# Normalising the attention weights before they are transposed, in a fused attention, gated-layer and expert kernel

## What is computed

```python
scores = scale * np.matmul(q, k.transpose(0, 1, 3, 2))
kth = np.partition(scores, -32, axis=-1)[..., -32:-31]
scores = np.where(scores >= kth, scores, -1e9)
scores = scores - np.max(scores, axis=-1, keepdims=True)
attn = np.exp(scores)
attn = attn / (np.sum(attn, axis=-1, keepdims=True) + 1e-09)
x = (attn @ v) as rows of 8 heads * 64            # 1152 x 512
rms = np.sqrt(np.mean(x * x, axis=-1, keepdims=True) + 1e-06)
xn = x / rms * rms_g
g = xn @ w_gate                                   # 512 x 1536
h = (g * sigmoid(g) * (xn @ w_val)) @ w_out       # 1536 x 512
# then top-1 of 8 experts by h @ gate, each expert relu(h @ w1) @ w2, times its probability
```

## Time and profile before

| what | value |
|---|---|
| median of 3 runs | 645.54 us (644.76 to 645.86) |
| the profiled execution, its own time | 645.43 us |
| its span, first to last instruction | 643.5 us |
| PE busy | 615.3 us |
| DVE busy | 411.7 us |
| ACT busy | 327.1 us |
| POOL busy | 264.4 us |
| mean granted TensorE clock | 0.994 |

### The profile page before, as it was taken

The page is one execution under the profiler, slowest core; times in us unless marked ns, Lnnn a source line. Parts: engine busy times, 40 slices in busy tenths (PEclk is TensorE's granted clock), DMA queues, the critical chain, the costliest instruction groups (busy, mean ns, idle before and its releaser), DMA issues.

```text
span 643.5 us, 11169 instructions
## 1 busy us (share of the span) xinstructions
PE 615.3 (96%) x3954; PEld 475.0 (74%) x3954; DVE 411.7 (64%) x912; ACT 327.1 (51%) x713; POOL 264.4 (41%) x366
## 2 busy tenths in 40 slices
PE   6789989999999999999999999999999999999994
PEld 5465765775765866766766766757589999999994
DVE  4999999898998997997997997902011111011110
ACT  4777876766766766766756757743111111111100
POOL 1876774364465464553654554542310110111101
PEclk9899999999999999999999999999999999999998
DMA  9998800000000000000000000000595876766501
GB/s 241 250 380 303 221 3 0 18 18 2 17 18 1 18 18 2 16 18 2 18 18 2 1 18 2 1 17 1 197 381 175 281 251 214 281 205 248 173 2 39
DMA packets 55182, 65.45 MB, mean 102 GB/s; under 512 B 32282, under 2 KB 32282, under 8 KB 55132
## 3 DMA queue, kind: packets, MB, share of 16 engines
q1 hardware_dynamic: 53388, 60.05, 29.5%
q0 software_dynamic: 1744, 4.76, 2.0%
HBM read 52.89 MB, written 12.30 MB: 101 GB/s over the span
## 4 chain that ended last, share of the span: by engine, by line
PE 85%; DVE 7%; ACT 2%; issue 2%; POOL 1%; DMA 1%; SPq 0%; POOLq 0%; ACTq 0%; DVEq 0%
PE ps L570 14%; PE ps L861 11%; PE ps L847 11%; PE ps L524 7%; PE ps L530 7%; PE ps L525 7%; PE ps L505 6%; PE ps L478 5%; PE ps L463 4%; PE ps L489 4%; DVE w_top L1360 2%; DVE m L1354 2%; PE ps L698 1%; DVE w_top L1347 1%; PE ps L872 1%
## 5 line engine op out<-in xcount | busy, mean ns | idle before, releaser
L1548 POOL TENSOR_TENSOR s_ring<-s_ring,z_pair 128x576 f32<-128x576 f32 x72 | 101.0, 1424 | 62.2 <-ACT z_pair L1055 62.2
L1360 DVE MATCH_REPLACE8 w_top<-m,w_top 128x576 f32<-128x576 f32 x144 | 105.9, 743 | 0.0
L1354 DVE MAX8 m<-w_top 128x8 f32<-128x576 f32 x144 | 101.7, 748 | 0.0
L570 PE MATMUL ps<-wo_space,hid 128*128 128x512 f32 x216 | 100.7, 593 | 0.8 <-issue 0.8
L524 PE MATMUL ps<-w_parts,x_hi 128*128 128x512 f32 x196 | 81.7, 417 | 0.0
L525 PE MATMUL ps<-w_parts,x_hi 128*128 128x512 f32 x196 | 77.4, 395 | 0.0
L861 PE MATMUL ps<-arena,w_loads 128*128 128x168 f32 x512 | 75.8, 307 | 0.5 <-issue 0.5
L1571 POOL DMA_INDIRECT out_rows<-arena,s_ring x16 | 15.1, 944 | 147.0 <-DVE arena L1384 144.6
L847 PE MATMUL ps<-arena,w_loads 128*128 128x168 f32 x512 | 74.3, 306 | 0.6 <-ACT arena L920 0.6
L847 PEld LDWEIGHTS ps<-arena,w_loads 128*128 128x128 f32 x512 | 73.3, 190 | 0.9 <-ACT arena L920 0.9
L861 PEld LDWEIGHTS ps<-arena,w_loads 128*128 128x128 f32 x512 | 73.2, 190 | 0.6 <-issue 0.6
(11 more groups left out here) (142 smaller groups left out, 885.8 us busy)
## 6 DMA issues: line engine op xcount, KB each, us to landing
w_loads<-in_moe_w SPq DMA_DIRECT2D x16, 2048.0 KB, 9.0
dispatched_rows<-drow SPq DMA_DIRECT2D x18, 260.0 KB, 6.7
w_loads<-in_moe_w_gate SPq DMA_DIRECT2D x3, 1024.0 KB, 5.9
w_loads<-in_moe_w_val SPq DMA_DIRECT2D x3, 1024.0 KB, 8.1
wo_space<-in_moe_w_out SPq DMA_DIRECT2D x1, 3072.0 KB, 12.1
arena<-dispatched_rows SPq DMA_DIRECT2D x8, 341.2 KB
out_rows<-drow SPq DMA_DIRECT2D x9, 256.0 KB, 5.4
q_space<-in_q SPq DMA_DIRECT2D x8, 256.0 KB, 4.2
```

The source lines that it names most:

```text
L570: last = mm(blk[0], hid[:, c * P:(c + 1) * P], wo_s[:, c, :], start=(c == 0), stop=(c == CF - 1))
L1354: vec.max(m8[:, 2 * (n % 2) + a, i, :], w_top[:, a, :]).then_inc(s["top_step"], 1)
L1360: vec.match_replace(w_top[:, a, :], m8[:, 2 * (n % 2) + a, i, :], w_top[:, a, :], NEG).then_inc(s["top_step"], 1)
L1548: gp.tensor_tensor(row, row, z_pair[:, a, :], ALU.subtract).then_inc(s["lowered"], 1)
```

## The change

The exponentials are divided by their row sum before PE transposes them. For that each half of a group gets its own two POOL instructions on one value per row (`divide`: add the epsilon, raise to the power -1), followed by an ACT pass over the 576 exponentials (`shares`), and PE's `turn_probs` waits for `shared` in place of `masked`. The product with the values then is x's columns already. So `x_hi` and `x_lo` are made from `oT` (the last pair's `x_hi` straight from PSUM, `last_columns`), the eight transposes around `xrow` with their copies and scalings go, and one turn of four transposes (`turn_columns`) takes their place, which feeds the sum of squares alone. The order on ACT and POOL changes with it: both `probs` of a group stand together in most slots, and from group 11 on (`early_marks`) the marks are made at the end of the slot before, ahead of that slot's last layer work.

```diff
             turned("rk", due(n, ALPHA, RANK))
+            turned("sq", due(n, ALPHA, XB))
             turned("q", next_tile(n))
...
-            turned("xa", due(n, GAMMA, XA))
-            turned("xn", due(n, GAMMA, XA))
...
             def turn_probs(g, a):
-                pe.wait_ge(s["masked"], 2 * g + a + 1)
+                pe.wait_ge(s["shared"], 2 * g + a + 1)
...
             def block_low(t, w_hi, bank):
-                pe.wait_ge(s["t_free"], use["xn", t] + 1)
+                pe.wait_ge(s["x_lo_set"], t + 1)
...
+            def turn_columns(t):
+                pe.wait_ge(s["o_copied"], HP * (t + 1))
+                turn(use["sq", t], lambda c: oT[:, c, :])
...
-                nc.scalar.activation(sqr, xrow[:], ACT.Square,
-                                     scale=float(DM) ** -0.5, accum_out=ssq[:, 0:1]).then_inc(s["x_sum"], 1)
+                nc.scalar.activation(sqr, tb, ACT.Square,
+                                     scale=float(DM) ** -0.5, accum_out=ssq[:, 0:1]).then_inc(s["t_free"], 1)
...
+            def last_columns(t):
+                act.wait_ge(s["pv_done"], H * (t + 1))
+                nc.scalar.activation(x_hi[:, (HP - 1) * P:HP * P], oT_ps, ACT.Copy,
+                                     scale=gain[:, HP - 1:HP]).then_inc(s["x_hi_set"], 1)
...
+            def shares(g, a):
+                act.wait_ge(s["share_set"], 2 * g + a + 1)
+                row = s_ring[:, g % SR, a, :]
+                nc.scalar.activation(row, row, ACT.Copy, scale=rden[:, g % 2, a:a + 1]).then_inc(s["shared"], 1)
...
+            def early_marks(g):
+                return g > FIRST + HP
...
+                if n + 1 <= NG and early_marks(n):
+                    marks(n, 0)
+                    marks(n, 1)
+                t = due(n, GAMMA, XA)
+                if t is not None and t > 0:
+                    columns(t, range(HP - 1))
+                dense(n, GAMMA)
...
+            def divide(g, a):
+                pool.wait_ge(s["masked"], 2 * g + a + 1)
+                gp.tensor_scalar(rden[:, g % 2, a:a + 1], den[:, g % 2, a:a + 1], EPS_SUM, None, ALU.add).then_inc(s["den_step"], 1)
+                pool.wait_ge(s["den_step"], 2 * g + a + 1)
+                gp.tensor_tensor(rden[:, g % 2, a:a + 1], rden[:, g % 2, a:a + 1], nones[:, 0:1], ALU.pow).then_inc(s["share_set"], 1)
...
                         gp.tensor_tensor(row, row, z_pair[:, a, :], ALU.subtract).then_inc(s["lowered"], 1)
+                    divide(g, 0)
+                    divide(g, 1)
+                if g > FIRST + HP and due(n - 1, GAMMA, V[2]) is not None:
+                    gate_by_value(due(n - 1, GAMMA, V[2]), 2)
```

More of the change, by code:

```diff
@@ L683, in dense @@
                     t = due(n, at, G[i])
[L684 to L688, removed]
+                    if t is not None and t > 0:
+                        pe.wait_ge(s["silu_done"], t * 3 + i)
                         ffn_block(t, (wg_hi, wg_lo), i, blk[1])
@@ L733, in _ @@
                     dense(n, ALPHA)
-                    turn_last_pair(n, t)
-                    if t > 0 and n + 1 < NG:
+                    for i in (4, 5):
+                        before = due(n, ALPHA, OUT[i][0])
+                        if before is not None:
+                            ffn_out(before, i)
+                    if t > 0:
+                        if n + 1 < NG:
+                            scores(n + 1)
+                        if probs:
+                            turn_columns(t)
+                            gate_high(t, 0)
+                            turn_probs(g, 0)
+                            gate_low(t, 0)
+                        else:
+                            gate_high(t, 0)
+                            turn_columns(t)
+                            gate_low(t, 0)
+                    else:
+                        pe.wait_ge(s["k1_copied"], KC)
+                        pe.wait_ge(s["w_lo_set"], LOW_ORDER.index(1) + 1)
+                        gate_high(0, 0)
+                        turn_columns(0)
                         scores(n + 1)
-                    if t > 0 and probs:
-                        gate_high(t, 0)
+                        gate_low(0, 0)
+                        first_block((wv_hi, wv_lo), 0, blk[0])
                         turn_probs(g, 0)
-                        gate_low(t, 0)
-                    else:
-                        dense(n, BETA)
-                        if t == 0:
-                            first_block((wv_hi, wv_lo), 0, blk[0])
-                        if probs:
-                            turn_probs(g, 0)
-                        if t == 0:
-                            first_block_end((wv_hi, wv_lo), 0, blk[0])
+                        first_block_end((wv_hi, wv_lo), 0, blk[0])
                     turn_out(n)
@@ L1136, in _ @@
                         probs(g, 1)
+                        shares(g, 0)
+                        shares(g, 1)
                         turned_probs(g, 0)
@@ L1142, in _ @@
                         turned_probs(g, 2)
-                    t = due(n, GAMMA, XA)
-                    if t is not None:
-                        raw_rows(t)
                     if n == HP:
+                        columns(0, range(HP - 1))
                         score_rows(n + 1, 1)
@@ L1154, in _ @@
                             keys(1, i, blk[i % 2]).then_inc(s["k1_copied"], 1)
-                    dense(n, GAMMA)
                 else:
+                    hidden_first = due(n, ALPHA, HID[1]) is not None
                     if 0 <= g - 1 < NG:
                         out_columns(g - 1)
-                    if here:
+                    if here and not early_marks(g):
                         marks(g, 0)
@@ L1165, in _ @@
                         probs(g, 0)
-                    dense(n, ALPHA)
+                    if hidden_first:
+                        dense(n, ALPHA)
+                    if here:
+                        probs(g, 1)
+                        shares(g, 0)
+                    if not hidden_first:
+                        dense(n, ALPHA)
                     out_rows(n)
+                    if here:
+                        shares(g, 1)
                     if n + 1 < NG:
                         score_rows(n + 1, 0)
-                    if here:
-                        probs(g, 1)
                     around = here and (n == FIRST + 1 or due(n, BETA, G[1]) is not None)
@@ L1349, in _ @@
                         beside(n - 1, GAMMA)
+                        low_part(n, True)
                 for i in (1, 2):
```

145 lines of the change are left out of this document (31 added, 114 removed).

## The result

The changed kernel takes **663.48 us** (median of 4 runs, 662.54 to 664.15) where the kernel before takes 645.15 beside it (4 runs): 1.028 times as long, 95% interval 1.027 to 1.030. Forecast were 652.8 us, with a range of 643.8 to 657.3. The profiled execution has a span of 661.3 us against 643.5.

A forecast was written before the change was run, and what follows sets the result against it. DVE's search was taken to pace slots up to about 8, PE's stream those from slot 9. Early losses +11.55, later tiles -2.7 and first and last turn slots -1.6 sum to +7.25: 652.8 us, range 643.8 to 657.3.

The forecast's parts named there:

- the chain from marks to PE: Slots 6 and 7: PE can transpose 5.45 us after the marks start, where it came at 3.80 before.
- the loss in slot 4t+7: Tiles from slot 12 on: later shares there take back 0.55 of the 0.8 us saved per tile.
- Slots 1 to 5: Start, paced by DVE: passes and divide waits delay score copies, making DVE 2.4 us late; bounds 0 and 3.3.
- Slots 6 to 11: Slots without early marks: PE stalls of 1.1 to 1.95 us each for the longer chain, sum 8.55.
- copy effect: Slots 9 and 10: second half's transposes wait for a pt copy queued later on ACT, 0.55 each, 1.1 us.
- the credit: Slots 6 and 7, where DVE paces: PE has some slack, so 0.5 us is taken off the loss.
- Tiles from slot 12 on: Six later tiles with early marks: 0.45 us saved each, -2.7; bounds 0.8 saved and 0.3 lost per tile.
- the walk (0.25): Slot 4t+7 traced step by step: share ready at 272.85, PE there at 272.3, so 0.55 of 0.8 lost.
- full cover: Tiles from slot 12 on: the upper bound, with the whole 0.8 us saved per tile.
- The last turn slot gives 0.8.: First and last turn slots: PE's shorter stream saves 0.8 us each, -1.6 together.
- The rival "worse": Slot 4t+7 walk short by 0.5, tiles lose 0.3, 657.2 us; or TensorE's clock falls, a stretch costing 1.5; chance 0.14.
- The faster rival: Stalls of slots 6 to 8 and the start cost nothing, later tiles keep 0.8: 642.3 us; chance 0.18.

The follow-up runs named there:

- run with the score copies first: Changed kernel, but in slots 1 to 4 ACT copies both halves of the next group's scores ahead of the two shares passes: 665.82 us, ratio 1.030.
- no division, copy first: Changed kernel without POOL's divide and ACT's pass, third value block copied to xrow ahead of the early marks in slots 4t+7: 641.23 us, ratio 0.994.
- the runs with filling: Changed kernel with useless matmuls in PE's waits: slots 7 and 35, 663.31 us, with fewer matmuls 663.55; slots 1 and 8 filled too, 660.32.

## Why the prediction was wrong

Right were the direction, the mechanism and the prices: the chain from marks to PE (5.49 for 5.45), the pass (0.773), the divide, the loss in slot 4t+7 (0.42 to 0.53, forecast 0.55), the end of the stalls at slot 12, and a tile of 46.73 us (forecast 46.4). Four terms were mis-sized, all to the same side, and so the sum left the range.

- **"Slots 1 to 5", 2.4 us, bounds 0 and 3.3.** It measured 5.6. Two steps of it failed: "Over slots 3 and 4 that is 4.5", and "I let ACT's idle time absorb 0.9". The copy that DVE waits for is that of slot 4. Before, the marks of slot 4 start at 50.30 and the copy at 57.66, 7.36 later. The marks before, and then marks to copy now:

```profile
50.30 1.44 ACT L1055 ACTIVATE z_pair<-s_ring,nbias 128x576 f32<-128x576 f32 x2 [0.38 <-POOL nbias L1534]
```

```profile
53.94 1.47 ACT L1022 ACTIVATE z_pair<-s_ring,nbias 128x576 f32<-128x576 f32 x2
...
62.38 0.77 ACT L896 ACTIVATE pt<-ps 128x512 f32<-128x512 f32 x2 [1.59 <-PE ps L488]
63.03 0.98 ACT L995 ACTIVATE x_hi<-oT,gain 128x128 fp32r<-128x128 f32 x3
63.91 0.64 ACT L896 ACTIVATE s_ring<-ps 128x576 f32<-128x576 f32 x1
```

That is 9.97, or 2.61 more where 2.25 was forecast, and nothing was absorbed. The marks themselves start 4.27 later, counted from DVE's first search, where the walk had 2.25 for slot 3 alone: each slot's marks follow PE's values of the slot before, and PE waits for the new pass in slots 1, 3 and 4 (3.62, 1.63 and 1.36 us; before 1.39 in slot 1 and none in slots 3 and 4). The forecast priced ACT's queue and put PE's own waits here at nothing. 4.27 + 2.61 - 1.2 of cover makes DVE 5.7 late. A part is the clock near 30 us: the two kernels without the division have the same code up to slot 6, and the one with 0.91 in 20 to 60 us lost 1.14 us in slot 2, the one with 0.96 nothing. The run with the score copies first shows that the queue isn't the only way in: there DVE waited 5.02 us for tile 0's columns, which end the same chain.
- **"Slots 6 to 11", 9.15 us with the copy effect and the credit.** It measured 11.8. Of this 1.6 is the fall of the clock in slot 7, behind a wait of 1.82 us, which the prediction had as a rival with the right price (1.5) but not in the sum. The credit of 0.5 wasn't there, and slot 6 lost 0.4 more than forecast. `x_lo`, 2.3 us longer in slot 5 where DVE paces, is a term that the forecast put at nothing, and may be that 0.4. Slot 6 lost 1.76 both in the run where it took 2.30 and in the division on the kernel before, where it is short. Without the division slots 6 and 7 lose 1.5 us with it; beside PE's own stalls no run shows more than these 0.3.
- **"Tiles from slot 12 on", 0.45 saved each.** It measured 0.12: the 0.8 was 0.66 (no division, copy first), and 0.5 went to slot 4t+7. I had taken the middle between the walk (0.25) and full cover; the walk was nearer. The step that failed is that choice, as no row spoke for full cover.
- **"The last turn slot gives 0.8."** From slot 35 on 2.2 us were lost. Slot 35 has no scores of a next group, 1.24 us of PE's stream, so PE came that much earlier to a chain that was no shorter, waited 1.92, and the clock fell behind it. This is read from the timelines; of it the runs with filling show the clock's part, 0.6. The prediction took the last slots for ordinary ones.

The rival "worse" had the clock, but its 657.2 was also too low. The faster rival (0.18) failed as argued: the delay of the start was not hidden, as it reached DVE itself.

## What to carry to other kernels

Work moved from behind a product to ahead of it costs its whole chain in every slot where nothing else is late, and it also delays what is queued behind it on its engine; walk the first and last slots of a pipeline apart, as their cover differs. A stall priced at 1 to 2 us may cost another 1.6 through the clock, and where several gaps stand in a row, closing one can move the fall to the next: it did in one of two runs with slots 7 and 35 filled. Moving a wait-bound step earlier in an in-order queue (the early marks) pays only if what stands behind it isn't waited for: look at what is queued behind it before looking at what it releases.

## What the hardware showed that I had not expected

DVE's instruction with both large operands in SBUF, started beside a POOL subtraction of SBUF tensors, ended only when that had ended: 1.5 to 1.6 us instead of 0.35, and the same shape with one operand in PSUM, fully beside the same subtraction, takes 0.35 (maximum of all 36: 0.352). The Trainium skill, SBUF — State Buffer, in "SBUF: two separate sides", says that DVE with two SBUF inputs and a GpSimd instruction that reads SBUF take turns on a shared pair of ports, and that the later one blocks for the other's whole instruction; the traces agree. The change moved `x_lo`'s first operand from PSUM to SBUF, so the rule spoke against it, and the prediction had left it out. In the two kernels without the division it stands beside 1.5 us lost in slots 6 and 7, out of the 5.3 that the shorter PE stream gives; that all of the 1.5 is its doing is not shown.
